# GpSimd takes half of the next expert's first-layer weight split, and the table load and dense halves move

## The reference

```python
def _attn_ref(q, k, v, centroids):            # 2 batches, 8 heads, 768 positions, 64 wide, 16 clusters
    ...                                        # nearest centroid of each query and key
    mask = q_assign[:, :, :, None] == k_assign[:, :, None, :]
    scores = np.where(mask, scale * q @ k.T, -1e9)
    return softmax(scores) @ v

def _moe_ref(x, w_gate, w_output_gate, w1, w2):   # 8 experts, 512 -> 1024 -> 512
    e_idx = np.argmax(x @ w_gate, axis=1)
    ...
    for e in range(E):
        mask = e_idx == e
        h = np.maximum(x[mask] @ w1[e], 0.0)
        out[mask] = gate_w[mask, None] * eom[mask, e, None] * (h @ w2[e])

def _moe2_ref(x, w_in, w_out):                # 512 -> 2048 -> 512
    h = x @ w_in
    g = h * (1.0 / (1.0 + np.exp(-1.702 * h)))
    return g @ w_out
```

## Time and profile before

| | us |
|---|---|
| median of 3 runs | 763.48 (762.52 to 766.73) |
| the profiled execution | 761.84 |
| its span | 760.1 |
| PE busy | 734.6, 97% of the span |
| DVE, ACT, POOL busy | 421.8, 381.0, 168.8 |

### The profile page before, as it was taken

The page is one execution under the profiler, slowest core; times in us unless marked ns, Lnnn a source line. Parts: engine busy times, 40 slices in busy tenths (PEclk is TensorE's granted clock), DMA queues, the critical chain, the costliest instruction groups (busy, mean ns, idle before and its releaser), DMA issues.

```text
span 760.1 us, 11527 instructions
## 1 busy us (share of the span) xinstructions
PE 734.6 (97%) x4013; PEld 626.1 (82%) x4013; DVE 421.8 (55%) x788; ACT 381.0 (50%) x722; POOL 168.8 (22%) x249
## 2 busy tenths in 40 slices
PE   7989999999999998999999999999999999999996
PEld 5788999988989986788888888778888888888884
DVE  5678887889879877756465655444122212131211
ACT  3677887877878864766666665533011101010101
POOL 5334424343863961000000000005202000020002
PEclk9999999999999999999999999999999999999998
DMA  7885364553727338847454742320001000010001
GB/s 152 194 196 125 74 149 108 139 126 88 180 78 207 126 150 277 319 170 263 164 188 149 250 170 94 129 93 1 0 1 56 0 1 1 0 57 1 0 1 55
DMA packets 60157, 86.13 MB, mean 113 GB/s; under 512 B 31552, under 2 KB 33600, under 8 KB 59584
## 3 DMA queue, kind: packets, MB, share of 16 engines
q1 hardware_dynamic: 53872, 74.69, 34.1%
q0 software_dynamic: 2352, 6.31, 2.2%
q10 hardware_dynamic: 3872, 4.36, 1.8%
HBM read 55.97 MB, written 8.92 MB: 85 GB/s over the span
## 4 chain that ended last, share of the span: by engine, by line
PE 81%; DVE 5%; SPq 4%; DMA 3%; POOL 3%; ACT 2%; issue 2%; ACTq 0%; DVEq 0%; POOLq 0%
PE ps L1026 17%; PE ps L728 11%; PE ps L807 6%; PE ps L1042 6%; PE ps L1043 5%; PE ps L1044 5%; PE ps L954 4%; PE ps L941 4%; PE ps L943 4%; PE ps L942 4%; PE ps L955 4%; PE ps L956 4%; SPq L413 3%; PE ps L783 3%; PE ps L779 3%; PE ps L794 2%
## 5 line engine op out<-in xcount | busy, mean ns | idle before, releaser
L1327 ACT ACTIVATE g<-ps 128x512 f32<-128x512 f32 x48 | 28.7, 598 | 205.6 <-PE ps L1026 203.5
L1736 DVE CAST gt_h<-g 128x512 fp32r<-128x512 f32 x48 | 20.9, 436 | 181.7 <-ACT g L1327 174.8
L1457 DVE TENSOR_TENSOR pt_l<-ps,pt_h 128x384 fp32r<-128x384 f32 x192 | 97.9, 550 | 32.8 <-ACT pt_h L1152 32.1
L1413 DVE TENSOR_REDUCE nmax<-ps 128x1 f32<-128x768 f32 x96 | 90.8, 947 | 5.2 <-PE ps L783 5.2
L1152 ACT CAST pt_h<-ps 128x384 fp32r<-128x384 f32 x192 | 84.9, 486 | 15.9 <-PE ps L728 15.9
L1128 ACT ACTIVATE probs<-ps,nmax 128x768 f32<-128x768 f32 x96 | 88.3, 920 | 6.6 <-DVE nmax L1413 6.6
L728 PE MATMUL ps<-ident,probs 128*128 128x128 f32 x576 | 83.6, 276 | 2.8 <-ACT probs L1128 1.9
L728 PEld LDWEIGHTS ps<-ident,probs 128*128 128x128 f32 x576 | 65.7, 140 | 12.5 <-DVE pt_l L1457 6.6
L1026 PE MATMUL ps<-x2t_h,wl 128*128 128x512 f32 x192 | 74.8, 389 | 0.0
L1026 PE MATMUL ps<-x2t_h,wh 128*128 128x512 f32 x192 | 74.7, 389 | 0.0
L1026 PE MATMUL ps<-x2t_l,wh 128*128 128x512 f32 x192 | 74.7, 389 | 0.0
(11 more groups left out here) (217 smaller groups left out, 1492.6 us busy)
## 6 DMA issues: line engine op xcount, KB each, us to landing
raw<-in_moe_w SPq DMA_DIRECT2D x32, 1024.0 KB, 7.1
ka<-hi_t SPq DMA_DIRECT2D x32, 192.0 KB, 4.0
raw<-in_moe_w_in SPq DMA_DIRECT2D x4, 1024.0 KB, 5.8
raw<-in_moe_w_out SPq DMA_DIRECT2D x4, 1024.0 KB, 6.7
xg<-xs ACTq DMA_DIRECT2D x15, 256.0 KB, 4.0
qn<-in_q SPq DMA_DIRECT2D x16, 192.0 KB, 3.6
vn<-in_v SPq DMA_DIRECT2D x8, 384.0 KB, 4.5
qa<-hi_t SPq DMA_DIRECT2D x16, 192.0 KB, 3.4
```

The lines of the kernel that those rows point to most:

```text
L1413: nc.vector.reduce_max(nmax[:, s % 4:s % 4 + 1], halves(score_bank(s)), AX.XY, negate=True).then_inc(m_ready, 1)
L1457: nc.vector.tensor_tensor(pt_l[g % 2][at_p], ps[:, 4 + half, 0:GQ].rearrange("p (c n) -> p c n", c=GT), pt_h[g % 2][at_p].bitcast(F32), AL ...
```

## The change

1. POOL gets a loop behind its last scatter. For e = 2 to 8 it waits for the second DMA of expert e's first-layer weights and splits pieces 2 and 3: a cast and a subtraction each. ACT and DVE split pieces 0 and 1 alone, also for an expert with a single tile. Expert 1 stays as it was.
2. POOL then splits two pieces of expert 8's second half (`w_in` columns of f = 8 to 15); ACT and DVE do the other two behind the loop.
3. PE waits for POOL's pieces on new semaphores, `w1_own` and `w2_own`; the counts of the old ones are made to fit.
4. ACT's load of the gelu table moves from the end of the expert loop to its start, behind the second piece of expert 1.
5. Behind the loop PE puts `tile_transpose` first and `hidden_transpose(last, 1)` ahead of `down(last, E - 1, 2)`; the half of dense column f = 1 is no longer done early, the whole column comes later. ACT and DVE do the last tile's `high` and `low` ahead of the splits.

```diff
@@ POOL, behind place_rows
+            for e in range(2, E + 1):
+                for i in (2, 3):
+                    pool.wait_ge(s_w[e % 2][1], 16 * (e // 2) + 16)
+                    nc.gpsimd.tensor_copy(half_at(wh, e % 2, i), half_at(raw, e % 2, i)).then_inc(w1_step, 1)
+                    pool.wait_ge(w1_step, 2 * (e - 2) + i - 1)
+                    nc.gpsimd.tensor_tensor(half_at(wl, e % 2, i), half_at(raw, e % 2, i), half_at(wh, e % 2, i).bitcast(F32), ALU.subtract).then_inc(w1_own, 1)
+            for i in (1, 3):
+                pool.wait_ge(s_w[E % 2][2 + i // 2], 16 * (E // 2) + 16)
+                ...
@@ PE, hidden
-                        pe.wait_ge(w1_lo if e else w0_lo, 4 * (e - 1 if e else 0) + c + 1)
+                        if e > 1 and c > 1:
+                            pe.wait_ge(w1_own, 2 * (e - 2) + c - 1)
+                        else:
+                            pe.wait_ge(w1_lo if e else w0_lo, first_count(e, c) if e else c + 1)
@@ PE, behind the loop
+            tile_transpose(total)
             down(last, E - 1, 0)
-            tile_transpose(total)
+            hidden_transpose(last, 1)
             down(last, E - 1, 2)
-            hidden_transpose(last, 1)
...
                     dense(0, 0, 2)
-                    dense(1, 0, 2)
                     down(last, E - 1, 4)
@@ ACT, ahead of the loop
             split_first(1, 1)
+            nc.scalar.activation(warm[:, 1:2], credit[:, 0:1], ACT.Gelu_apprx_sigmoid)
             tile_high(1)
@@ ACT, expert_tile (DVE likewise)
-                if k < 2:
+                if k == 0:
                     split(whose, 2)
...
-                for i in range(4):
+                for i in range(2):
                     split_first(e + 1, i)
@@ ACT, behind the loop (DVE likewise with low and split_second)
+            high(last, 1)
             split_second(E, 0)
             split_second(E, 2)
-            high(last, 1)
-            split_second(E, 1)
-            split_second(E, 3)
-
-            nc.scalar.activation(warm[:, 1:2], credit[:, 0:1], ACT.Gelu_apprx_sigmoid)
```

More of the change, by code:

```diff
@@ L301, in clustered_attention_moe_mlp @@
         w2_lo = sem("w2_lo")
+        w1_step = sem("w1_step")
+        w1_own = sem("w1_own")
+        w2_step = sem("w2_step")
+        w2_own = sem("w2_own")
         xg_in = sem("xg_in")
@@ L375, in expert_loop, with first_count, second_count @@
                         eng.reg_add(counter, counter, 1)
+        def first_count(e, i):
+            return i + 1 if e == 1 else 2 * e + i + 1
+        def second_count(e, i):
+            return 4 * (e - 1) + i + 1 if e <= E else 4 * (E - 1) + 2 + i + 1
         def piece_at(bufs, u, r):
@@ L705, in _ @@
                 place_rows(t)
+            for e in range(2, E + 1):
[6 more added lines that the diff above has]
+                pool.wait_ge(s_w[E % 2][2 + i // 2], 16 * (E // 2) + 16)
+                nc.gpsimd.tensor_copy(half_at(wh, E % 2, 4 + i), half_at(raw, E % 2, 4 + i)).then_inc(w2_step, 1)
+                pool.wait_ge(w2_step, i // 2 + 1)
+                nc.gpsimd.tensor_tensor(half_at(wl, E % 2, 4 + i), half_at(raw, E % 2, 4 + i), half_at(wh, E % 2, 4 + i).bitcast(F32), ALU.subtract).then_inc(w2_own, 1)
             pool.wait_ge(g_dense, 1)
@@ L1022, in dense @@
                         if m == 0 and c == 2 and f % 8 == 0:
-                            pe.wait_ge(w2_lo, 4 * (E - 1) + 2 + f // 4)
+                            pe.wait_ge(w2_own if f else w2_lo, 2 if f else second_count(E, 1))
                         w = slice((c % 2) * FF + f * P, (c % 2) * FF + (f + 1) * P)
@@ L1036, in dense_down @@
                     if m == 0 and f % 2 == 0:
-                        pe.wait_ge(w1_lo if f < 8 else w2_lo, 4 * E + f % 8 // 2 + 1)
+                        pe.wait_ge(w1_lo if f < 8 else w2_lo, (first_count if f < 8 else second_count)(E + 1, f % 8 // 2))
                     slot = 2 + f // 8
@@ L1062, in mlp_group @@
                     wait_apart(pe, x2l_done, total)
-                    pe.wait_ge(w1_lo, 4 * E)
+                    pe.wait_ge(w1_lo, first_count(E, 1))
+                    pe.wait_ge(w1_own, 2 * (E - 1))
                 if m == NMG - 1:
@@ L1072, in mlp_group @@
                 for f in range(1, FC2):
-                    dense(f, 0 if m or f > 1 else 2)
+                    dense(f)
                     if f == 1 and m == 0:
@@ L1635, in split_first @@
             def split_first(e, i):
-                dve.wait_ge(w1_hi, 4 * (e - 1) + i + 1)
+                dve.wait_ge(w1_hi, first_count(e, i))
                 nc.vector.tensor_tensor(half_at(wl, e % 2, i), half_at(raw, e % 2, i), half_at(wh, e % 2, i).bitcast(F32), ALU.subtract).then_inc(w1_lo, 1)
             def split_second(e, i, turn=None):
-                dve.wait_ge(w2_hi, 4 * (e - 1) + (i if turn is None else turn) + 1)
+                dve.wait_ge(w2_hi, second_count(e, i if turn is None else turn))
                 nc.vector.tensor_tensor(
@@ L1725, in _ @@
             row = row_at(last + 1)
+            low(last, 1)
             split_second(E, 0, 0)
             split_second(E, 2, 1)
-            low(last, 1)
-            split_second(E, 1, 2)
-            split_second(E, 3, 3)
             for m in range(NMG):
```

## The result

The changed kernel takes 776.15 us (median of 4 runs, 774.82 to 777.88). The kernel before, run beside it, takes 764.18 (4 runs, 762.52 to 766.73): ratio 1.016, 95% interval 1.0129 to 1.019. It is slower, as forecast, but by 12 us where 7.8 were forecast, and just above the forecast range (its upper end is 776). The profiled execution took 774.9, its span 773.1, 13.0 over before.

What follows compares the result with a forecast made beforehand. PE was taken to bound the expert loop. Blocking losses of 10.0 us, less 2.2 at the dense step, plus 0 for the table load, made 7.8 slower: 771.3 us, likeliest case 767 to 776, whole range 761.5 to 776.

Steps and rivals of the forecast that it cites:

- What bounds the kernel: Expert loop: PE bounds it, waiting 0.3 us in all from 320 to 460 us; little to win there.
- Blocking by whole instructions, in turns: DVE's two-SBUF-input splits and POOL's instructions alternate whole in the expert loop: 10.0 us lost; chance 0.68.
- The first rival: No blocking: POOL and DVE run side by side; gains 0.9 at expert 2, 2.2 at dense step: 760.4 us; chance 0.17.
- the second: DVE is held once, then both its splits precede POOL's next instruction: +2.1 us, 765.6 us; chance 0.13.
- The seven terms: Losses where DVE's splits meet POOL's pieces, experts 2 to 7 and the dense weights: 10.0 us in all.
- Expert 5: Its pieces' collision, a tie as close as 0.1 us: 0.7 us lost if DVE is first, 3.1 if POOL's cast.
- Expert 3: Its pieces' collision: a whole POOL subtraction of 2.4 us falls between DVE's two splits; 2.6 us lost.
- What is not hidden is DVE: Tile k = 0: DVE's last split pair stands right ahead of xt_l, with 0.3 us slack before PE's hidden.
- The dense step: Behind the expert loop: the ht_l wait goes and the first gelu comes sooner; gain 2.2 us.
- The table load: ACT's load of 1.28 us hides in idle time ahead of tile_high(1) at its new place: cost 0, otherwise 1.5.

Runs made afterwards that it cites:

- Experiments 4 and 8: Changed kernel with memsets replacing POOL's casts and subtractions: 758.72 us, ratio 0.9958; changed kernel with POOL's pieces split in quarters: 765.9 us, ratio 1.0052.
- after_again: The changed kernel measured once more, unaltered, against the kernel before: 771.48 us, ratio 1.0149.
- table_back: The changed kernel with ACT's gelu table load back at its old place behind the expert loop: 773.12 us, ratio 1.0153 to the kernel before.
- w1_only: The kernel before with only POOL's splitting of first-layer pieces 2 and 3 for experts 2 to 8 added: 774.44 us against 762.25, ratio 1.0156.
- experiment 7: Same run as table_back: the changed kernel with ACT's gelu table load back behind the expert loop: 773.12 us, ratio 1.0153.
- experiment 1: Same run as w1_only: the kernel before with only POOL's splitting of first-layer pieces added: 774.44 us against 762.25, ratio 1.0156.
- late_again: The kernel late_pool measured once more, on the chip of the quartered version: 759.36 us, ratio 0.9966 to the kernel before.
- late_pool: Changed kernel; for experts 3 to 8 POOL starts after DVE's second-layer splits of the expert in front, for expert 2 does one piece: 758.61 us, ratio 0.9948.

## Why the prediction was right and wrong

What each place costs, by how much later PE stands behind it than in the trace of before:

| place | forecast | measured | of it at half clock |
|---|---|---|---|
| up to expert 1's first layer | 0 | 1.15 | 1.3 |
| first layer of expert 2 | 0.8 | 2.7 | 1.6 |
| expert 3 | 2.6 | 1.0 | |
| expert 4 | 1.0 | 1.15 | |
| expert 5 | 0.7 | 3.85 | 1.6 |
| expert 6 | 1.6 | 1.65 | |
| expert 7 | 1.4 | 1.2 | |
| `w_in` | 1.9 | 2.5 | |
| step to the dense stage | -2.2 | -2.3 | |
| sum | 7.8 | 12.9 | 4.5 |

Without the clock 8.4 us are left, against 7.8. The row of an expert is that of its pieces on POOL: "expert 4" is the collision in tile 0 of expert 3, and so on.

- **What bounds the kernel**, and that only DVE's pair ahead of `xt_l` can hurt: right. PE waits six times for `xt_l`, and once for `wl` in expert 2.
- **Blocking by whole instructions, in turns**: right, from one collision of 0.46 us. The first rival (no blocking) falls with the pair of 5.03, the second (held once) too: both splits of a pair are held there and in tile 0 of expert 3 (1.9 and 2.1 us). Experiments 4 and 8 show it from two further sides.
- **The seven terms** (expert 2 to `w_in`): 14.1 measured, less 3.2 of clock, 10.9 against 10.0. The same sum, less the clock, is 8.6 in `after_again`, 12.6 in `table_back` and 9.9 in `w1_only`, so the forecast lies in the middle of what one execution or another shows. The single terms were less good than the sum. Expert 5 was called a tie as close as 0.1 us and taken at 0.7; the cast was first, and it was 2.25 without the clock (the other side was 3.1). Expert 3 was taken at 2.6 since a whole subtraction was to fall between the splits. POOL was a piece further than I had it: its last subtraction began at 332.2, DVE's pair at 333.0, and with POOL done the second split was free. In `table_back` the subtraction did fall between the splits, and expert 3 cost 2.4 without the clock. So each place has several outcomes, and the execution chooses. That the two misses cancel in the first trace is luck; the wide range was the honest part.
- **Restarts**: the first matmul behind a pause is followed after 0.33 rather than 0.23 us. About 0.1 at each place, 0.7 in all (an estimate from these steps), was not counted; it is in the 10.9.
- **The failed step** is "What is not hidden is DVE", which counts a pause of PE at its length. Behind two of the loop's pauses PE's clock went to its half level, and that cost 3.2 us which no term had; the fall at 292 cost 1.3 more. The clock is thus 4.5 of the 5.1 us by which the trace misses the forecast. In the second measurement, with two falls in the profiled run, the kernel was 9.3 over and not 12. Nothing in the trace of before shows it in the loop, where PE never paused for so long. It had one such fall in the attention stage, near 18.6 us, behind a pause of PE from 14.60 to 17.34: the granted clock from 15 to 25 us is 0.83. I used it only as a mean over the execution, 0.995, and that hides such a stretch.
- **Before the loop**: I forecast nothing ahead of 300 us and PE was 1.15 us late there. PE no longer waits for `ht_l` at 290.26, and waits for the tile's tokens instead, until 292.36, with a fall of the clock behind it. The load of the table is not the cause (experiment 7), POOL's loop as such is not either (experiment 1 has a wait of 0.6 there, not 2.0). `late_again` has the same wait, 2.2, with no fall behind it, and PE gains 0.2 there on the kernel before. So it is the fall behind it that costs. The wait is not tied to the edit either: `late_pool`, the same kernel, waited 0.5 there on another chip. PE's row at that place, in `late_pool`, then in `late_again`:

```profile
291.67 0.66 PE L753 MATMUL ps<-ident,xg 128*128 128x128 f32 x4 [0.54 <-DMA xg<-xs]
...
291.83 0.66 PE L753 MATMUL ps<-ident,xg 128*128 128x128 f32 x4 [2.16 <-DMA xg<-xs]
```

  Both start at almost the same time, when the tokens are there; what differs is whether the pause ahead comes in one piece. Why it does stays open.
- **The dense step**: right in size and in mechanism. PE waits 0.44 for the `w_out` split where it waited 1.65, the wait for `ht_l` is gone, and `dense_down(0)` follows the first gelu by 3.4 as forecast.
- **The table load**: right. It takes 1.28 again and ACT still has 2.69 idle behind it, ahead of `tile_high(1)`:

```profile
288.87 1.28 ACT L1289 ACT_TABLE_LOAD   x1
290.17 0.20 ACT L1289 ACTIVATE warm<-credit 128x1 f32<-128x1 f32 x1
293.05 0.59 ACT L1233 CAST xt_h<-ps 128x512 fp32r<-128x512 f32 x1 [2.69 <-PE ps L751]
```

## What to carry to other kernels

Before work goes to an idle GpSimd, look at where it falls beside DVE operations with two SBUF inputs, and which of these stand just ahead of what TensorE waits for: make it start behind those (here that, with one piece given back, turned +1.6% into -0.3 to -0.5%), or cut its instructions short (+0.5%). A start that waits for a DMA's landing fell at different places beside DVE's pair from one execution of the changed kernel to the next; a start that waits for DVE's own progress fell at the same place in both traces. Ask also what the move can earn: where TensorE was the engine that bound the loop, it earned 0.1 us over six experts. Where a change makes TensorE pause in a stage in which it never paused, price the pauses at more than their length (here 1.3 to 1.6 us for each fall, and not every pause had one).

## What the runs showed of the hardware

- POOL's cast or subtraction and DVE's two-input subtraction exclude each other for whole instructions: a split of 1.22 us came to as much as 3.4, POOL's cast of 1.04 to 2.06, its subtraction of 2.39 to 3.26. With memsets of the same size on POOL all stayed as they were.
- TensorE's clock fell to its half level behind some of its pauses of 2.4 to 3.6 us in a stage that is otherwise full (start to start: 289.95 to 292.36, 318.24 to 321.83, 389.24 to 391.60 in the first trace of the changed kernel) and not behind others as long (472.02 to 474.62 there, 317.94 to 321.06 in `after_again`). Each fall cost 1.3 to 1.6 us.
- A subtraction of a quarter of the columns took POOL 0.74 us where the whole took 2.39, a cast 0.40 where the whole took 1.04: a straight line through either pair leaves some 0.2 us for each instruction (an estimate).
